# Sliding-window attention ahead of an expert layer: a longer pipeline (four stages instead of three between the scores and their use), a second transposed-probability buffer, a third value buffer, and another order on DVE

## The chip, the cores and the metric

One core of a Trainium2 chip. The time is the device time of one execution, in microseconds (us). Engines: PE (TensorE, matrix products), DVE (VectorE), ACT (ScalarE), POOL (GpSimd), SP (SyncE, which here only issues DMAs). Each works its own instructions in order and meets the others at semaphores.

## The reference

```python
B, H, S, D = 4, 8, 576, 64            # q, k, v
mask = (rel >= 0) & (rel < 64)        # each query sees itself and 63 keys before it
attn = softmax(where(mask, q @ k.T / 8, -1e9))
x = (attn @ v)  ->  (B*S, H*D) = (2304, 512)
P = exp(x @ w_gate - max); 8 rounds of row and column normalisation   # 2304 x 8
out = sum over 8 experts e of P[:, e] * (relu(x @ w1[e]) @ w2[e])       # w1 512x1024, w2 1024x512
```

## The kernel before, in words

**Attention** works on 16 pairs of heads (`NP`), numbered p. Of a pair, 9 blocks of 64 queries are treated at once, each against 128 keys (its own 64 and the 64 before). The stages of a pair, with the short names used below:

- S(p), PE, `scores` L343: 36 small products into the PSUM area `ps_s`.
- own(p), ACT, `own` L601: copies the own-block half of the scores to `sc`, one of three buffers.
- merge(p), DVE, `merge`: L923 puts the previous-block half over it where the mask says so, and lets PE have `ps_s` again (`scores_taken`); L926 takes the row maximum.
- shift(p), POOL, L825: subtracts the maximum. exp(p), ACT, L596.
- soften(p), DVE, L931 and L933: row sums and their reciprocals. weigh(p), POOL, L833: `probs`, two buffers.
- T(p), PE, `transpose` L355, into the PSUM area `ps_t`. turned(p), DVE, L917: masks it into `p_t`, one buffer.
- v_shift(p), ACT, L607: builds the "block before" rows of V in `v_win`, two buffers. M(p), PE, `mix` L366.
- x_copy(p), ACT, L614 and L617: copies x out of PSUM, and for p < 8 rounds parts of it to `xv_hi`. x_part_rests(p), DVE, L941: the rounding rest `xv_lo`.

The order of all of it is written out by hand. In turn p of the loop PE runs S(p), M(p-3), T(p-2); DVE turned(p-3), merge(p), soften(p-1), x_part_rests(p-3); ACT exp(p-1), own(p), x_copy(p-3), v_shift(p-2); POOL shift(p), weigh(p-1), and in some turns a piece of preparation for the expert layer (`w1_first_rest`, `sums_first`, `sums_last`, `w1_rest`, `x_sum`). ACT has two such pieces: `w1_first` and `w1_split`.

**After the loop** come four first-layer products of expert 0, `plain(0)` to `plain(3)`, each of 12 matmuls (L467 to L469), with the last mixes and transposes between them, then the gate products (L375). Before the first S(0) PE multiplies zeros 12 times (L531).

**The expert layer** is 96 steps of seven-product 2x2 block multiplication for the first layer (L445 to L449) and 2 x 6 x 3 matmuls for the second (L486 to L488), with DVE, ACT and POOL splitting operands into a rounded part and a rest. The change leaves it as it is.

Of the kernel before, what the change touches and what calls it, by code (L numbers as in the profile page):

```python
# [12 lines left out]
P = 128  # L13
# [17 lines left out]
QKR = 3  # L31
WARM = 12
# [34 lines left out]
def build(nc, qk, v, w_gate, w1, w2, consts, out):  # L67
    with ExitStack() as ctx:
# [17 lines left out]
        p1 = sb(ctx, "p1", [P, HT])  # L86
        u2 = sb(ctx, "u2", [P, HT])
        u3 = sb(ctx, "u3", [P, HT])
        u4 = sb(ctx, "u4", [P, HT])

        wg = sb(ctx, "wg", [P, KT, GC])
        logits = sb(ctx, "logits", [P, NT, E])
        prob = sb(ctx, "prob", [P, NT, E])
# [3 lines left out]
        max_diag = sb(ctx, "max_diag", [P, P])  # L97
# [6 lines left out]
        with ExitStack() as att:  # L104
            qk_buf = sb(att, "qk_buf", [P, QKR, QK])
            v_win = sb(att, "v_win", [P, 2, QB, P])
            sc = sb(att, "sc", [P, SCR, QB, WINDOW])
# [4 lines left out]
            soft_inv = sb(att, "soft_inv", [P, SCR, QB])  # L112
        warm = p_t[:].rearrange("p i c -> p (i c)").bitcast(mybir.dt.bfloat16)
# [5 lines left out]
        w2_lo += [sb(ctx, "w2_lo1", [P, 2, DM], F32R)]  # L119

# [8 lines left out]
        ps_t = ps[:, 1536:1536 + QB * P].rearrange("p (i c) -> p i c", i=QB)  # L129
        x_at = 7 * 512 - 5 * WINDOW  # L130
# [20 lines left out]
        v_loaded = [sem(f"v_loaded{i}") for i in range(2)]  # L151
# [112 lines left out]
        def _(sp):  # L264
# [6 lines left out]
            def load_v(p):  # L271

                if p >= 2:
                    sp.wait_ge(x_done, p - 1)
                sp.dma_start(v_win[WINDOW:P, p % 2, :, :], v[p]).then_inc(v_loaded[p % 2], 16)
# [15 lines left out]
            load_v(0)  # L291
            load_w1(0, 0, 0)
            load_v(1)
            for p in range(NP):
                if p + QKR < NP:
                    load_qk(p + QKR)
                if p >= 3:
                    load_v(p - 1)
                if p == 3:
                    sp.dma_start(wg[:], w_gate).then_inc(gate_loaded, 16)  # L300
                if p == 3:
# [32 lines left out]
        def _(pe):  # L334
            def scores(p):
                pe.wait_ge(qk_loaded[p % QKR], (p // QKR + 1) * 16)
                wait(pe, scores_taken, p)
                for i in range(QB):

                    at = 0 if i else WINDOW  # L340
                    for h in range(2):
                        c = slice(h * D, (h + 1) * D)
                        last = nc.tensor.matmul(ps_s[c, i, at:KEYS],  # L343
                                                qk_buf[c, p % QKR, S + i * WINDOW:S + (i + 1) * WINDOW],
                                                qk_buf[c, p % QKR, max(i - 1, 0) * WINDOW:(i + 1) * WINDOW],
                                                start=True, stop=True)
                last.then_inc(scores_done, 1)
# [184 lines left out]
            pe.wait_ge(pads_set, 2)  # L532
# [34 lines left out]
        def _(act):  # L567
# [25 lines left out]
            def exp(p):  # L593
                act.wait_ge(shifted, p + 1)
                e = sc[:, p % SCR, :, :]
                nc.scalar.activation(e, e, ACT.Exp, scale=float(D) ** -0.5).then_inc(exp_done, 1)  # L596

            def own(p):
                act.wait_ge(scores_done, p + 1)
                wait(act, probs_ready, p - SCR + 1)  # L600
                nc.scalar.copy(sc[:, p % SCR, :, :], ps_s[:, :, WINDOW:KEYS]).then_inc(own_taken, 1)  # L601

            def v_shift(p):

                act.wait_ge(v_loaded[p % 2], (p // 2 + 1) * 16)
                wait(act, x_done, p - 1)
                nc.scalar.copy(v_win[0:WINDOW, p % 2, 1:QB, :], v_win[WINDOW:P, p % 2, 0:QB - 1, :])\  # L607
                  .then_inc(v_shifted, 1)
# [11 lines left out]
            def p1_copy(n, slot):  # L620
                act.wait_ge(prod_done, n * PRODUCTS + (P1 + 1 - PRODUCTS))
                wait(act, u2_done, n + -1)
                nc.scalar.copy(p1[:], bank[slot]).then_inc(p1_out, 1)
# [77 lines left out]
            for p in range(NP):  # L701
# [9 lines left out]
                if p == 9:  # L711
                    w1_split(1, 1, 0)
                if p == 14:
                    x_split(0, P6)
            x_split(0, P7)
            v_shift(NP - 2)
            x_copy(NP - 3)
            exp(NP - 1)
            plain_relu(0)
            w2_split(16, 0, 0)  # L720
            x_split(0, P5)
            v_shift(NP - 1)
            plain_relu(1)
            x_copy(NP - 2)
            x_split(0, P4)
            plain_relu(2)
            x_copy(NP - 1)
            plain_relu(3)
# [22 lines left out]
        def _(pool):  # L751
# [76 lines left out]
            def weigh(p):  # L828
# [4 lines left out]
                nc.gpsimd.tensor_tensor(probs[:, p % 2, :, :, :], sc[:, k, :, :].unsqueeze(2).to_broadcast(both),  # L833
# [6 lines left out]
            for p in range(NP):  # L840
# [3 lines left out]
                if p in (5, 6):  # L844
                    w1_first_rest(p - 5)
                if p == 7:
                    sums_first(1, 16)
                if p == 8:
                    sums_last(1, 1)
                if p == 9:  # L850
                    x_sum(0, T1)
                if p == 10:
                    w1_rest(1, 1, 0, 2)
                if p == 11:
                    w1_rest(1, 1, 2, 4)
                if p == 12:
                    x_sum(0, T2)
                if p == 13:
                    w1_rest(1, 1, 4, 7)
                if p == 14:  # L860
                    x_sum(0, T3)
            weigh(NP - 1)
            x_rest(0, P6, 1)
            w2_rest(0, 0)
# [48 lines left out]
        def _(dve):  # L913
            def turned(p):
                dve.wait_ge(transposed, p + 1)
                wait(dve, x_done, p)
                nc.vector.tensor_tensor(p_t[:], ps_t, seen.unsqueeze(1).to_broadcast([P, QB, P]), ALU.mult)\  # L917
                  .then_inc(p_t_ready, 1)

            def merge(p):  # L920
                k = p % SCR
                dve.wait_ge(own_taken, p + 1)
                nc.vector.copy_predicated(sc[:, k, :, :], take_before.unsqueeze(1).to_broadcast([P, QB, WINDOW]),  # L923
                                          ps_s[:, :, 0:WINDOW]).then_inc(scores_taken, 1)
                dve.wait_ge(scores_taken, p + 1)
                nc.vector.tensor_reduce(row_max[:, k, :], sc[:, k, :, :], AX_X, ALU.max).then_inc(max_done, 1)  # L926

            def soften(p):
                k = p % SCR
                dve.wait_ge(exp_done, p + 1)  # L930
                nc.vector.tensor_reduce(soft_sum[:, k, :], sc[:, k, :, :], AX_X, ALU.add).then_inc(sum_done, 1)  # L931
# [19 lines left out]
            def add_u2(n, slot):  # L951
                dve.wait_ge(prod_done, n * PRODUCTS + (P6 + 1 - PRODUCTS))
                dve.wait_ge(p1_out, n)
                nc.vector.tensor_tensor(u2[:], bank[1 - slot], p1[:], ALU.add).then_inc(u2_done, 1)  # L954

            def add_u3(n, slot):
                dve.wait_ge(prod_done, n * PRODUCTS + (P7 + 1 - PRODUCTS))
                dve.wait_ge(u2_done, n)
                nc.vector.tensor_tensor(u3[:], bank[1 - slot], u2[:], ALU.add).then_inc(u3_done, 1)

            def add_c22(n, slot):
                dve.wait_ge(prod_done, n * PRODUCTS + (P5 + 1 - PRODUCTS))
                nc.vector.tensor_tensor(u4[:], bank[slot], u2[:], ALU.add).then_inc(u4_done, 1)  # L963
                dve.wait_ge(u3_done, n)
                dve.wait_ge(u4_done, n)
                nc.vector.tensor_tensor(bank[slot], bank[slot], u3[:], ALU.add).then_inc(c_done, 1)

            def add_c21(n, slot):
                dve.wait_ge(prod_done, n * PRODUCTS + (P4 + 1 - PRODUCTS))
                nc.vector.tensor_tensor(bank[1 - slot], bank[1 - slot], u2[:], ALU.add).then_inc(c_done, 1)  # L970

            def add_c12(n, slot):
                dve.wait_ge(prod_done, n * PRODUCTS + (P3 + 1 - PRODUCTS))
                nc.vector.tensor_tensor(bank[slot], bank[slot], u4[:], ALU.add).then_inc(c_done, 1)  # L974
# [106 lines left out]
            nc.vector.memset(ps_s[:, 0, 0:WINDOW], NEG).then_inc(pads_set, 1)  # L1081
            dve.wait_ge(const_loaded, 16)
            for p in range(NP):
                if p >= 3:
                    turned(p - 3)
                merge(p)
                if p:
                    soften(p - 1)
                if p >= 3:
                    x_part_rests(p - 3)  # L1090
            turned(NP - 3)
            soften(NP - 1)
# [76 lines left out]
```

## Time and profile before

| | us |
|---|---|
| median of 3 runs | 1604.66 (1604.3 to 1604.78) |
| the profiled execution | 1606.06 |
| its span, first to last instruction | 1604.2 |
| PE busy, share of the span | 1583.3 (99%) |
| DVE, ACT, POOL busy | 694.2, 544.8, 990.4 |
| first gate product on PE | 100.98 after the span's start |
| 16 loads of Q and K, 576 KB each, to landing | 6.4 (median) |
| 16 loads of V, 288 KB each, to landing | 4.3 (median) |

The profiled execution took 1.86 us more than its span (what lies around it) and 1.40 us more than the median. A busy PE in this table need not be working at its peak; whether it is held up is seen in its idle time and in what ended it.

### The profile page before, as it was taken

How to read it: one execution, taken by the hardware profiler on the slowest of the kernel's cores; microseconds unless marked ns; L12 is line 12 of the kernel's file. 1: busy time of each engine (PE TensorE's matmuls, PEld its weight loads, DVE VectorE, ACT ScalarE, POOL GpSimd, SP SyncE). 2: the span in 40 equal slices, each digit the busy share in tenths (PEclk: the TensorE clock that was granted, in tenths of full speed). 3: DMA queues.
4: the chain of work that ended last, by engine and by line, in shares of the span. 5: the costliest groups of instructions: out<-in, count | busy, mean ns of one | idle time of the engine just before them, and what ended most of it. 6: DMA issues, size and time to landing. Idle time of an engine off the chain costs nothing.

```text
span 1604.2 us, 24055 instructions
## 1 busy us (share of the span) xinstructions
PE 1583.3 (99%) x8886; PEld 1420.8 (89%) x8886; DVE 694.2 (43%) x1261; ACT 544.8 (34%) x785; POOL 990.4 (62%) x642
## 2 busy tenths in 40 slices
PE   7899999999999999999999999999999999999999
PEld 6789888989899888989989898998989889898988
DVE  6744543443443434434434434434344344344343
ACT  4643242323333342333323233333323333332331
POOL 4985656556565976656565565878556565655652
PEclk9999999999999999999999999999999999999999
DMA  7621212121211213121121212113121212212111
GB/s 218 177 73 67 79 54 79 53 79 52 78 62 69 78 52 119 53 79 61 70 78 52 78 52 78 60 71 118 53 79 53 78 57 73 78 52 78 52 65 39
DMA packets 34159, 120.44 MB, mean 75 GB/s; under 512 B 3904, under 2 KB 4160, under 8 KB 34112
## 3 DMA queue, kind: packets, MB, share of 16 engines
q1 hardware_dynamic: 34112, 119.80, 21.9%
q8 instruction: 31, 0.51, 0.1%
q14 instruction: 16, 0.13, 0.0%
HBM read 115.06 MB, written 4.72 MB: 75 GB/s over the span
## 4 chain that ended last, share of the span: by engine, by line
PE 94%; POOL 4%; issue 1%; DVE 1%; ACT 0%; POOLq 0%; DVEq 0%
PE ps L488 17%; PE ps L487 17%; PE ps L486 16%; PE ps L449 14%; PE ps L445 14%; PE ps L447 14%; POOL probs L833 2%; POOL sc L825 1%; PE ps L343 0%; POOL t_raw L814 0%; PE ps L531 0%; PE ps L355 0%; POOL w_lo L791 0%; DVE x_raw L990 0%; PE ps L366 0%
## 5 line engine op out<-in xcount | busy, mean ns | idle before, releaser
L791 POOL TENSOR_TENSOR w_lo<-w_raw,w_hi 128x1792 fp32r<-128x1792 f32 (+2 forms) x97 | 386.5, 3985 | 540.2 <-ACT w_hi L571 540.2
L626 ACT ACTIVATE h_hi<-ps 128x384 fp32r<-128x384 f32 x384 | 186.5, 492 | 872.3 <-DVE ps L974 434.0
L488 PE MATMUL ps<-w_hi,h_lo 128*128 128x512 f32 x1152 | 454.1, 394 | 0.0
L487 PE MATMUL ps<-w_lo,h_hi 128*128 128x512 f32 x1152 | 453.1, 393 | 0.0
L486 PE MATMUL ps<-w_hi,h_hi 128*128 128x512 f32 x1152 | 451.5, 392 | 0.0
L449 PE MATMUL ps<-xv_hi,w_lo 128*128 128x384 f32 x1330 | 445.8, 335 | 0.0
L445 PE MATMUL ps<-xv_hi,w_hi 128*128 128x384 f32 x1330 | 444.8, 334 | 0.7 <-DVE h_lo L948 0.7
L447 PE MATMUL ps<-xv_lo,w_hi 128*128 128x384 f32 x1330 | 444.3, 334 | 0.0
L948 DVE SCALAR_TENSOR_TENSOR h_lo<-ps,h_hi 128x384 fp32r<-128x384 f32 x384 | 205.9, 556 | 266.8 <-ACT h_hi L626 257.9
L445 PEld LDWEIGHTS ps<-xv_hi,w_hi 128*128 128x128 f32 x1330 | 249.7, 188 | 17.9 <-DVE h_lo L948 2.0
L447 PEld LDWEIGHTS ps<-xv_lo,w_hi 128*128 128x128 f32 x1330 | 249.7, 188 | 16.7
L488 PEld LDWEIGHTS ps<-w_hi,h_lo 128*128 128x128 f32 x1152 | 216.0, 187 | 48.0
L449 PEld LDWEIGHTS ps<-xv_hi,w_lo 128*128 128x128 f32 x1330 | 249.7, 188 | 0.0
L487 PEld LDWEIGHTS ps<-w_lo,h_hi 128*128 128x128 f32 x1152 | 216.0, 188 | 34.4
L486 PEld LDWEIGHTS ps<-w_hi,h_hi 128*128 128x128 f32 x1152 | 216.2, 188 | 34.0
L798 POOL TENSOR_TENSOR w_lo<-w_raw,w_hi 128x1024 fp32r<-128x1024 f32 x96 | 231.0, 2406 | 14.0 <-ACT w_hi L582 14.0
L571 ACT CAST w_hi<-w_raw 128x1792 fp32r<-128x1792 f32 x95 | 161.5, 1700 | 5.6 <-POOL w_raw L773 5.5
L974 DVE TENSOR_TENSOR ps<-ps,u 128x384 f32<-128x384 f32 x95 | 53.8, 567 | 234.7 <-PE ps L449 234.7
L954 DVE TENSOR_TENSOR u<-ps,p 128x384 f32<-128x384 f32 x95 | 53.0, 558 | 158.3 <-PE ps L449 158.3
L990 DVE SCALAR_TENSOR_TENSOR x_raw<-ps,prob,x_raw 128x512 f32<-128x512 f32 x126 | 93.9, 748 | 59.0 <-PE ps L488 58.1
L963 DVE TENSOR_TENSOR u<-ps,u 128x384 f32<-128x384 f32 x95 | 53.0, 558 | 137.8 <-PE ps L449 137.8
L582 ACT CAST w_hi<-w_raw 128x1024 fp32r<-128x1024 f32 x96 | 99.7, 1039 | 0.0
(87 smaller groups left out, 961.4 us busy)
## 6 DMA issues: line engine op xcount, KB each, us to landing
w_raw<-w SPq DMA_DIRECT2D x192, 512.0 KB, 3.9
qk_buf<-qk SPq DMA_DIRECT2D x16, 576.0 KB, 6.4
v_win<-v SPq DMA_DIRECT2D x16, 288.0 KB, 4.3
out<-x_raw SPq DMA_DIRECT2D x18, 256.0 KB, 4.3
const_sb<-consts SPq DMA_DIRECT2D x1, 176.0 KB, 3.6
wg<-w_gate SPq DMA_DIRECT2D x1, 64.0 KB, 5.1
```

The lines of the kernel that those rows point to most:

```text
L445: nc.tensor.matmul(o, w1_hi[:, slot, c], xv_hi[:, at, kk, :], start=(opens and kk == 0), stop=False, skip_group_check=not opens)
L447: nc.tensor.matmul(o, w1_hi[:, slot, c], xv_lo[:, at, kk, :], start=False, stop=False, skip_group_check=not opens)
L449: last = nc.tensor.matmul(o, w1_lo[:, slot, c], xv_hi[:, at, kk, :], start=False, stop=(kk == 1), skip_group_check=not opens)
L486: nc.tensor.matmul(ps_y[t], h_hi[slot][:, f, c], w2_hi[slot][:, f, :], start=opens, stop=False)
L487: nc.tensor.matmul(ps_y[t], h_hi[slot][:, f, c], w2_lo[slot][:, f, :], start=False, stop=False)
L488: last = nc.tensor.matmul(ps_y[t], h_lo[slot][:, f, c], w2_hi[slot][:, f, :], start=False, stop=closes)
L571: nc.scalar.copy(w1_hi[:, slot, :], w1_raw[:, slot, BLK:RAW]).then_inc(w1_hi_ready, 1)
L582: nc.scalar.copy(w2_hi[slot][:].rearrange("p f d -> p (f d)"), w2_raw[:, slot, :])\
L626: nc.scalar.activation(h_hi[slot][:, f, half * HT:(half + 1) * HT], o, ACT.Relu)\
L791: last = nc.gpsimd.tensor_tensor(w1_lo[:, slot, c], w1_raw[:, slot, (lo + 1) * BLK:(hi + 1) * BLK], w1_hi[:, slot, c].bitcast(F32), ALU.su ...
L798: nc.gpsimd.tensor_tensor(w2_lo[slot][:].rearrange("p f d -> p (f d)"), w2_raw[:, slot, :], w2_hi[slot][:].rearrange("p f d -> p (f d)").b ...
L948: nc.vector.scalar_tensor_tensor(h_lo[slot][:, f, c], o, 0.0, h_hi[slot][:, f, c].bitcast(F32), ALU.max, ALU.subtract).then_inc(h_ready, 1)
```

## The change

- `v_win` gets three buffers (`VR`), and `load_v(p)` waits for M(p-3) in place of M(p-2).
- `p_t` gets a second buffer for odd pairs, `us`, which is the memory of `p1`, `u2`, `u3` of the expert layer, idle until then. turned(p) waits for M(p-2) in place of M(p-1).
- To make room, `sc` has two buffers of its own, and the third lies in a part of `w1_raw` that is unused until the expert layer. `logits`, `prob` and `max_diag` lie elsewhere. (In the trace `us` and `w_raw` then stand where `p_t` and `sc` stood.)
- S(1) goes to `ps_t`, so that it need not wait for merge(0); S(2) waits for merge(0), S(3) for merge(2).
- In turn p PE runs S(p), T(p-3), M(p-4). DVE runs soften(p-1), merge(p), turned(p-3), x_part_rests(p-4). ACT runs exp(p-1), own(p), v_shift(p-3), x_copy(p-4). One more mix and transpose lie behind the loop.
- The pieces for the expert layer sit one turn later or so: `w1_first` at turn 5, `w1_split` at 10; on POOL, turns 6 to 11, 12, 13 and 14, the third `x_sum` behind the loop. The load of w1 moves from the start to turn 3.

```diff
             def transpose / mix / attend (PE)
-                wait(pe, scores_taken, p)
+                wait(pe, scores_taken, {1: 0, 2: 1}.get(p, p))
-                        last = nc.tensor.matmul(ps_s[c, i, at:KEYS],
+                        last = nc.tensor.matmul(ps_of[p][c, i, at:KEYS],
...
                 if p < NP:
                     scores(p)
-                if p >= 3:
-
-                    wait(pe, x_taken, p - 3)
-                    wait(pe, x_part_lo, parts_in(p - 3))
-                    mix(p - 3)
-                if 2 <= p < NP + 2:
-                    transpose(p - 2)
+                if 3 <= p < NP + 3:
+                    transpose(p - 3)
+                if p >= 4:
+                    wait(pe, x_taken, p - 4)
+                    wait(pe, x_part_lo, parts_in(p - 4))
+                    mix(p - 4)
...
             plain(0)
             attend(NP)
+            attend(NP + 1)
             plain(1)
-            attend(NP + 1)
+            attend(NP + 2)
             plain(2)
-            attend(NP + 2)
+            attend(NP + 3)
             plain(3)
```

```diff
                 dve.wait_ge(transposed, p + 1)
-                wait(dve, x_done, p)
-                nc.vector.tensor_tensor(p_t[:], ps_t, ...)
+                wait(dve, x_done, p - 1)
+                nc.vector.tensor_tensor(p_ts[p % 2], ps_t, ...)
...
             for p in range(NP):
+                if p:
+                    soften(p - 1)
+                merge(p)
                 if p >= 3:
                     turned(p - 3)
-                merge(p)
-                if p:
-                    soften(p - 1)
-                if p >= 3:
-                    x_part_rests(p - 3)
-            turned(NP - 3)
+                if p >= 4:
+                    x_part_rests(p - 4)
             soften(NP - 1)
+            turned(NP - 3)
```

```diff
             def load_v(p):
-                if p >= 2:
-                    sp.wait_ge(x_done, p - 1)
+                if p >= VR:
+                    sp.wait_ge(x_done, p - VR + 1)
...
                 own(p)
                 if p >= 3:
-                    x_copy(p - 3)
-                if p >= 2:
-                    v_shift(p - 2)
-                if p == 4:
+                    v_shift(p - 3)
+                if p >= 4:
+                    x_copy(p - 4)
+                if p == 5:
                     w1_first()
-                if p == 9:
+                if p == 10:
                     w1_split(1, 1, 0)
```

How PE's instructions stand at the start. Before, from S(2) (first two rows) to S(4):

```order
L343 MATMUL ps<-qk_buf 64x64 x2
L343 MATMUL ps<-qk_buf 64x128 x16
L355 MATMUL ps<-const_sb,probs 128x128 x9
L343 MATMUL ps<-qk_buf 64x64 x2
L343 MATMUL ps<-qk_buf 64x128 x16
L366 MATMUL ps<-p_t,v_win 64x64 x18
L355 MATMUL ps<-const_sb,probs 128x128 x9
L343 MATMUL ps<-qk_buf 64x64 x2
L343 MATMUL ps<-qk_buf 64x128 x16
```

In the changed kernel (L351 is S, L363 T, L374 M), from S(2) to S(5):

```order
L351 MATMUL ps<-qk_buf 64x64 x2
L351 MATMUL ps<-qk_buf 64x128 x16
L351 MATMUL ps<-qk_buf 64x64 x2
L351 MATMUL ps<-qk_buf 64x128 x16
L363 MATMUL ps<-const_sb,probs 128x128 x9
L351 MATMUL ps<-qk_buf 64x64 x2
L351 MATMUL ps<-qk_buf 64x128 x16
L363 MATMUL ps<-const_sb,probs 128x128 x9
L374 MATMUL ps<-p_t,v_win 64x64 x18
L351 MATMUL ps<-qk_buf 64x64 x2
L351 MATMUL ps<-qk_buf 64x128 x16
```

T(0) stood between S(2) and S(3) and now stands behind S(3); M(0) has moved from behind S(3) to behind S(4) and T(1).

DVE's turn 7 before, which is turned(4), merge(7), soften(6), x_part_rests(4), and the turned(5) that opens the next:

```order
L917 TENSOR_TENSOR p_t<-ps,const_sb 128x1152
L923 COPY_PREDICATED sc<-const_sb,ps 128x576
L926 TENSOR_REDUCE row_max<-sc 128x9
L931 TENSOR_REDUCE soft_sum<-sc 128x9
L933 RECIPROCAL soft_inv<-soft_sum 128x9
L941 TENSOR_TENSOR xv_lo<-ps,xv_hi 128x192
L917 TENSOR_TENSOR p_t<-ps,const_sb 128x1152
```

DVE's turn 8 in the changed kernel, which is soften(7), merge(8), turned(5), x_part_rests(4), and the sums that open the next:

```order
L940 TENSOR_REDUCE soft_sum<-sc 128x9
L942 RECIPROCAL soft_inv<-soft_sum 128x9
L932 COPY_PREDICATED w_raw<-const_sb,ps 128x576
L935 TENSOR_REDUCE row_max<-w_raw 128x9
L926 TENSOR_TENSOR us<-ps,const_sb 128x1152
L950 TENSOR_TENSOR xv_lo<-ps,xv_hi 128x192
L940 TENSOR_REDUCE soft_sum<-w_raw 128x9
```

The sums of the pair before stood behind the merge and now stand ahead of it; turned stood ahead of the merge and now stands behind it.

## Rows read from the trace of the kernel before

**Rows 1.** The chain that ended last, from 0 to 130 us, by line.
```profile
by line: POOL probs L833 21.0%; POOL sc L825 12.2%; issue 11.0%; PE ps L343 3.6%; POOL t_raw L814 3.4%; PE ps L445 3.1%; PE ps L531 3.1%; PE ps L486 3.1%; PE ps L449 3.0%; PE ps L447 2.9%; PE ps L488 2.9%; PE ps L487 2.8%; PE ps L355 2.7%; 
```

**Rows 2.** Windows: stretch and length, then each engine's busy us.
```profile
60.00:80.00 20.00, 17.16 (x323) 15.50 (x320) 15.45 (x23) 12.34 (x21) 18.02 (x12) 1.00 0.53 139
120.00:140.00 20.00, 20.00 (x103) 18.06 (x102) 9.71 (x23) 5.49 (x9) 9.83 (x7) 1.00 0.24 87
```

**Rows 3.** Waits of PE, 19 to 101 us: total us, times, longest.
```profile
PE ps L366 <- DVE p_t L917: 5.5, 8, 1.3
```

**Rows 4.** Timeline of PE: start, length, line, tiles, count, idle before.
```profile
14.69 2.08 PE L343 MATMUL ps<-qk_buf 64*64 64x64 f32 x36 [2.01 <-DVE sc L923]
...
19.88 2.08 PE L343 MATMUL ps<-qk_buf 64*64 64x64 f32 x36
21.89 1.27 PE L366 MATMUL ps<-p_t,v_win 128*64 128x64 f32 x36
23.09 1.20 PE L355 MATMUL ps<-const_sb,probs 128*128 128x128 f32 x9
24.22 2.08 PE L343 MATMUL ps<-qk_buf 64*64 64x64 f32 x36
...
80.29 2.08 PE L343 MATMUL ps<-qk_buf 64*64 64x64 f32 x36
...
85.07 0.42 PE L467 MATMUL ps<-xv_hi,w_hi 128*128 128x384 f32 x1
...
87.34 1.27 PE L366 MATMUL ps<-p_t,v_win 128*64 128x64 f32 x36
...
100.98 0.63 PE L375 MATMUL ps<-x_raw,wg 128*32 128x512 f32 x3
```

**Rows 5.** Timeline of all engines, 11 to 16 us: one round of the softmax stages.
```profile
11.32 1.15 POOL L825 TENSOR_TENSOR sc<-sc,row_max 128x576 f32<-128x576 f32 x1 [10.27 <-DVE row_max L926]
12.51 0.68 ACT L596 ACTIVATE sc<-sc 128x576 f32<-128x576 f32 x1 [2.96 <-POOL sc L825]
...
13.75 0.79 DVE L923 COPY_PREDICATED sc<-const_sb,ps 128x576 f32<-128x576 uint32 x1 [2.51 <-ACT sc L601]
14.58 0.75 DVE L926 TENSOR_REDUCE row_max<-sc 128x9 f32<-128x576 f32 x1
...
15.41 1.15 POOL L825 TENSOR_TENSOR sc<-sc,row_max 128x576 f32<-128x576 f32 x1 [2.94 <-DVE row_max L926]
```

**Rows 6.** Timeline of ACT and DVE, 89 to 91 us: exp(15) and its sums.
```profile
89.32 0.68 ACT L596 ACTIVATE sc<-sc 128x576 f32<-128x576 f32 x1
...
90.03 0.76 DVE L931 TENSOR_REDUCE soft_sum<-sc 128x9 f32<-128x576 f32 x1 [3.06 <-ACT sc L596]
```

**Rows 7.** Timeline of DVE, 24 to 27 us, without idle time between.
```profile
23.54 0.76 DVE L926 TENSOR_REDUCE row_max<-sc 128x9 f32<-128x576 f32 x1
24.21 0.74 DVE L931 TENSOR_REDUCE soft_sum<-sc 128x9 f32<-128x576 f32 x1
24.98 0.21 DVE L933 RECIPROCAL soft_inv<-soft_sum 128x9 f32<-128x9 f32 x1
25.11 0.76 DVE L941 TENSOR_TENSOR xv_lo<-ps,xv_hi 128x384 fp32r<-128x384 f32 x2
25.79 1.35 DVE L917 TENSOR_TENSOR p_t<-ps,const_sb 128x1152 f32<-128x1152 f32 x1
```

**Rows 8.** Timeline, 54 to 58 us: a weigh and an extra piece on POOL, `w1_split` on ACT.
```profile
55.22 2.12 POOL L833 TENSOR_TENSOR probs<-sc,soft_inv 128x1152 f32<-128x1152 f32 x1
56.02 1.69 ACT L571 CAST w_hi<-w_raw 128x1792 fp32r<-128x1792 f32 x1
...
57.29 1.82 POOL L814 TENSOR_TENSOR t_raw<-x_raw 128x768 f32<-128x768 f32 x1
```

**Rows 9.** Timeline of PE, 2 to 9 us: the zero products, then S(0).
```profile
2.14 4.02 PE L531 MATMUL ps<-p_t 128*128 128x384 bf16 x12 [2.14 <-DVE p_t L1079]
6.09 2.77 PE L343 MATMUL ps<-qk_buf 64*64 64x64 f32 x36
```

More of the change, by code:

```diff
@@ L31 @@
 QKR = 3
+VR = 3
 WARM = 12
@@ L85, in build @@
         w2_raw = sb(ctx, "w2_raw", [P, 2, 2 * DM])
[L86 to L89, printed above, removed]
+        us = sb(ctx, "us", [P, 4, HT])
+        p1, u2, u3, u4 = (us[:, i, :] for i in range(4))
         wg = sb(ctx, "wg", [P, KT, GC])
-        logits = sb(ctx, "logits", [P, NT, E])
-        prob = sb(ctx, "prob", [P, NT, E])
         col_part = sb(ctx, "col_part", [P, E])
@@ L112, in build @@
             soft_inv = sb(att, "soft_inv", [P, SCR, QB])
+        v_bufs = [v_win[:, i, :, :] for i in range(VR)]
+        p_ts = [p_t[:], us[:].rearrange("p r t -> p (r t)")[:, 0:QB * P].rearrange("p (i c) -> p i c", i=QB)]
+        sc_of = [sc[:, i, :, :] for i in range(SCR - 1)]
+        sc_of += [w1_raw[:, 0, 4 * BLK:4 * BLK + QB * WINDOW].rearrange("p (i c) -> p i c", i=QB)]
         warm = p_t[:].rearrange("p i c -> p (i c)").bitcast(mybir.dt.bfloat16)
@@ L119, in build @@
         w2_lo += [sb(ctx, "w2_lo1", [P, 2, DM], F32R)]
+        logits = sb(ctx, "logits", [P, NT, E])
+        prob = sb(ctx, "prob", [P, NT, E])
+        max_diag = sb(ctx, "max_diag", [P, P])
         take_before = const_sb[:, 0:WINDOW].bitcast(mybir.dt.uint32)
@@ L129, in build @@
         ps_t = ps[:, 1536:1536 + QB * P].rearrange("p (i c) -> p i c", i=QB)
+        ps_of = [ps_t if p == 1 else ps_s for p in range(NP)]
         x_at = 7 * 512 - 5 * WINDOW
@@ L150, in build @@
         qk_loaded = [sem(f"qk_loaded{i}") for i in range(QKR)]
-        v_loaded = [sem(f"v_loaded{i}") for i in range(2)]
+        v_loaded = [sem(f"v_loaded{i}") for i in range(VR)]
         v_shifted = sem("v_shifted")
@@ L296, in _ @@
                     load_qk(p + QKR)
-                if p >= 3:
+                if p < VR:
+                    load_v(p)
+                if p > VR:
                     load_v(p - 1)
@@ L365, in mix @@
                         c = slice(h * D, (h + 1) * D)
-                        last = nc.tensor.matmul(ps_x[c, i * WINDOW:(i + 1) * WINDOW], v_win[:, p % 2, i, c],
-                                                p_t[:, i, c], start=True, stop=True)
+                        last = nc.tensor.matmul(ps_x[c, i * WINDOW:(i + 1) * WINDOW], v_bufs[p % VR][:, i, c],
+                                                p_ts[p % 2][:, i, c], start=True, stop=True)
                 last.then_inc(x_done, 1)
@@ L600, in own @@
                 wait(act, probs_ready, p - SCR + 1)
-                nc.scalar.copy(sc[:, p % SCR, :, :], ps_s[:, :, WINDOW:KEYS]).then_inc(own_taken, 1)
+                nc.scalar.copy(sc_of[p % SCR], ps_of[p][:, :, WINDOW:KEYS]).then_inc(own_taken, 1)
             def v_shift(p):
-                act.wait_ge(v_loaded[p % 2], (p // 2 + 1) * 16)
-                wait(act, x_done, p - 1)
-                nc.scalar.copy(v_win[0:WINDOW, p % 2, 1:QB, :], v_win[WINDOW:P, p % 2, 0:QB - 1, :])\
+                act.wait_ge(v_loaded[p % VR], (p // VR + 1) * 16)
+                wait(act, x_done, p - VR + 1)
+                nc.scalar.copy(v_bufs[p % VR][0:WINDOW, 1:QB, :], v_bufs[p % VR][WINDOW:P, 0:QB - 1, :])\
                   .then_inc(v_shifted, 1)
@@ L705, in _ @@
                 if p >= 3:
-                    x_copy(p - 3)
-                if p >= 2:
-                    v_shift(p - 2)
-                if p == 4:
+                    v_shift(p - 3)
+                if p >= 4:
+                    x_copy(p - 4)
+                if p == 5:
                     w1_first()
-                if p == 9:
+                if p == 10:
                     w1_split(1, 1, 0)
-                if p == 14:
-                    x_split(0, P6)
-            x_split(0, P7)
+            v_shift(NP - 3)
+            exp(NP - 1)
+            plain_relu(0)
+            x_split(0, P6)
+            x_copy(NP - 4)
             v_shift(NP - 2)
             x_copy(NP - 3)
-            exp(NP - 1)
-            plain_relu(0)
+            plain_relu(1)
+            v_shift(NP - 1)
             w2_split(16, 0, 0)
+            x_split(0, P7)
+            x_copy(NP - 2)
             x_split(0, P5)
[L722 to L725, printed above, removed]
             plain_relu(2)
             x_copy(NP - 1)
+            x_split(0, P4)
             plain_relu(3)
@@ L843, in _ @@
                     weigh(p - 1)
-                if p in (5, 6):
-                    w1_first_rest(p - 5)
-                if p == 7:
+                if p in (6, 7):
+                    w1_first_rest(p - 6)
+                if p == 8:
                     sums_first(1, 16)
-                if p == 8:
+                if p == 9:
                     sums_last(1, 1)
-                if p == 9:
+                if p == 10:
                     x_sum(0, T1)
-                if p == 10:
+                if p == 11:
                     w1_rest(1, 1, 0, 2)
-                if p == 11:
+                if p == 12:
                     w1_rest(1, 1, 2, 4)
-                if p == 12:
-                    x_sum(0, T2)
                 if p == 13:
@@ L915, in turned @@
                 dve.wait_ge(transposed, p + 1)
-                wait(dve, x_done, p)
-                nc.vector.tensor_tensor(p_t[:], ps_t, seen.unsqueeze(1).to_broadcast([P, QB, P]), ALU.mult)\
+                wait(dve, x_done, p - 1)
+                nc.vector.tensor_tensor(p_ts[p % 2], ps_t, seen.unsqueeze(1).to_broadcast([P, QB, P]), ALU.mult)\
                   .then_inc(p_t_ready, 1)
@@ L930, in soften @@
                 dve.wait_ge(exp_done, p + 1)
-                nc.vector.tensor_reduce(soft_sum[:, k, :], sc[:, k, :, :], AX_X, ALU.add).then_inc(sum_done, 1)
+                nc.vector.tensor_reduce(soft_sum[:, k, :], sc_of[k], AX_X, ALU.add).then_inc(sum_done, 1)
                 dve.wait_ge(sum_done, p + 1)
@@ L953, in add_u2 @@
                 dve.wait_ge(p1_out, n)
-                nc.vector.tensor_tensor(u2[:], bank[1 - slot], p1[:], ALU.add).then_inc(u2_done, 1)
+                nc.vector.tensor_tensor(u2, bank[1 - slot], p1, ALU.add).then_inc(u2_done, 1)
             def add_u3(n, slot):
```

47 lines of the change are left out of this document (22 added, 25 removed).

## The prediction

> **What bounds the kernel now.** I read the windows first. In the expert layer PE is busy for 20.00 of 20 us; between 60 and 80 us, inside attention, for 17.16 [rows 2]. The change touches attention alone, so what it can move is the moment at which the gate products start, 100.98 us [rows 4]; PE is the limit from there on, and every microsecond gained or lost there should arrive at the end unchanged. Next the chain: over the first 130 us a third of it is weigh and shift on POOL (21.0% and 12.2%) [rows 1], so attention is bound by a round trip through several engines. The waits of PE say where that shows: 8 mixes waited 5.5 us in all for `p_t` [rows 3]. The timeline gives PE's own need: S starts at 19.88, M at 21.89, T at 23.09, the next S at 24.22, with no idle time [rows 4], so S costs 2.01, M 1.20, T 1.13, together 4.34 a pair. From S(4) at 24.22 to `plain(0)` at 85.07 there are 12 turns [rows 4] in 60.85 us, 5.07 each. At 4.34 they would take 52.1. So 8.8 us at most stand to be had there.
>
> **The change, part by part.**
>
> *Second `p_t`, third V, one more stage.* M(p-4) needs turned(p-4), made a whole turn earlier, and V stands in one of three buffers, so that its load starts a turn further ahead of its use. The 5.5 us of waits [rows 3] should go.
>
> *DVE's new order.* This is the part with a price. Soften(p-1) now stands ahead of merge(p), so a ring closes through every pair: shift, exp, sums, reciprocals, merge, maximum, next shift. From starts: shift to exp 12.51 - 11.32 = 1.19, merge to maximum 14.58 - 13.75 = 0.83, maximum to shift 15.41 - 14.58 = 0.83 [rows 5]; exp to sums 90.03 - 89.32 = 0.71 [rows 6]; sums to reciprocal 0.77, reciprocal to the next instruction 0.13 [rows 7]. Sum: 1.19 + 0.71 + 0.77 + 0.13 + 0.83 + 0.83 = **4.46 us a pair**. Before, own(p) alone lay between exp and merge and the ring took 15.41 - 11.32 = 4.09 [rows 5]. So the new floor is 4.46, set by the ring, not PE's 4.34. While shift and exp run, DVE is free from the end of the maximum for about 2.05 us (0.83 + 1.19 + 0.71 from its start, less the 24.21 - 23.54 = 0.67 that it holds DVE [rows 7]); turned (1.35) and the largest x_part_rests (0.68, the step from 25.11 to 25.79) fit with 2.03 [rows 7]. I cost them at nothing; were that cover gone, each 0.1 us would cost 0.4 over the four turns that have the large rests.
>
> *The start.* shift(0) starts at 11.32 as before. S(1) no longer waits for merge(0), which saves nothing: own(1) stands behind exp(0) on ACT anyway. shift(1) comes 0.4 later than the 15.41 of before. S(p+1) starts 0.72 ahead of shift(p) (14.69 against 15.41 [rows 4, 5]).
>
> *Extra pieces.* POOL needs shift and weigh, about 1.16 + 2.07 = 3.23, in a turn (57.29 - 55.22 = 2.07 [rows 8]). A piece of 1.82 us [rows 8] makes it 5.03 and so adds 0.57 to the ring. Four are of that length: turns 6, 10, 13 and 14 (the last delays only shift(15)). The two pairs of short sums (turns 8, 9), some 1.4 to 1.5 together, add 0.2 to 0.3 each. ACT's `w1_first` at turn 5, about 1.0, stands between x_copy(1) and exp(5), where ACT has some 0.7 to spare: 0.3. `w1_split`, 1.69 [rows 8], overlaps turn 10's POOL piece: nothing more. Up to shift(14): 3 x 0.57 + 0.45 + 0.3 = 2.4.
>
> So shift(14) at 11.32 + 14 x 4.46 + 2.4 = 76.2 and S(15) at 75.5, against 80.29 [rows 4]: 4.8 us earlier.
>
> *The end.* PE then has S(15), four T, five M (one more than before) and four `plain` at 2.2 (85.07 to 87.34 less its wait [rows 4]): 2.0 + 4.6 + 6.0 + 8.8 = 21.4. Shift(15) is at 76.2 + 5.0 = 81.2; turned(13) stands behind soften(15) and ends at 81.2 + 1.19 + 0.71 + 0.90 + 1.35 = 85.4, and T(14) waits for it 0.9 us, the M(12) before it ending at 84.5. M(15) waits for x_copy(14), which is behind `w2_split` on ACT, but that ends at about 93.8, ahead of PE at 94.4. The gate starts at 75.5 + 21.4 + 0.9 = 97.8, **3.2 us earlier**. POOL's last rests come 2.5 earlier and had slack. Loads: V is issued a turn or more ahead of need and lands in 4.3; Q and K have 11 us for 6.4.
>
> *A hole on PE.* S(2) ends near 12.9 (S(1) from 8.9, S(2) behind it), and T(0), which used to fill the hole, stands behind S(3), which needs merge(2): 11.32 + 2 x 4.46 - 0.72 = 19.5. PE stands still for 6.6 us, where before no hole after the zero products was above 2.01 [rows 4]. What idleness does to it can be seen at the start: the zero products of 384 columns took 4.02 / 12 = 0.335 us each [rows 9], while the 12 products of `plain(0)`, as wide, took 87.34 - 85.07 = 2.27, 0.19 each [rows 4]: the first is the 1.2 GHz level, the second the 2.4 GHz one (the clock column of the windows reads 1.00 throughout [rows 2], and it reads so early on too, so here the spacing must tell). S(0) took 2.77 [rows 9] against the 2.08 of later ones [rows 4], so it began at the low level and ended at the high one: at half speed for about 1.4 us, PE came up some 5.4 us after its first product.
>
> The Trainium skill ("TensorE: Matmul & The Clock Gate", section "What's actually happening") says that the slow level is the default and that idleness brings it back. The zero products agree; no row of before shows a fall after work. By that rule the hole costs the 1.5 us worked out below, without it nothing.
>
> Price if the level has fallen by S(3) and returns about 5.4 us later: S(3) takes almost double, some 3.8 and not 2.0, own(3), due at 22.0, waits to 23.3, and merge(3) comes 1.0 late. T(0) takes twice as long, PE runs half a microsecond behind the ring, so x_copy(1) and `w1_first` end later and exp(5) slips a further 0.5. Together 1.5. The bounds: 0 if it doesn't fall, and 1.8 more for each further S at the low level.
>
> **The forecast.** 1604.66 - 3.2 + 1.5 = **1603.0**. (Of the profiled execution, 1606.06 would become 1604.4; I apply the difference to the median.) A change under 0.2%, 3.2 us, can't be told from none by a measurement of this kernel.
>
> **The rivals.**
> - *PE keeps its clock*: 1604.66 - 3.2 = 1601.5. For it: 2 us holes did no harm. Against: this one is three times as long.
> - *The low level stays a little longer*, one or two more S: +1.8 to +3.6 on the forecast, 1604.8 to 1606.6, so no change.
> - *The low level stays for the whole loop*, slower than before. At half speed a pair needs up to 2 x 4.34 = 8.7 us against 4.46, over 12 turns 50 us: 1653. It decides if S, T and M with the holes of the first turns are too little activity to raise the clock. The trace shows it only kept by such work, never raised by it alone: the rise came behind twelve full-width products. Against it: at half speed PE would be busy without a break. The Trainium skill (same page, "Part 4: PE-mode transpose") says that transposes don't count as activity in the same way; no row here tests that.
> - *The ring is looser than I think*: the extra pieces hide, up to 2.4 us more gain, 1599.1 to 1601.
> - *The change does not do what it says* because the rest of the gain is lost at the end (ACT or POOL late for the last mixes): 1604 to 1605, the small change of the forecast again.
>
> **Chances.** Forecast 0.50 (own range 1602.0 to 1604.3); clock kept 0.24; low a little longer 0.12; low for good 0.05; looser ring 0.05; end eats it 0.04. Faster by over 0.2% (below 1601.45): half of clock kept and the looser ring and a little of the forecast, 0.20. Slower by over 0.2% (above 1607.9): 0.07. Within: 0.73. The range reaches from 1600.6 (part of the looser ring) to 1605.7 (part of the low level's further stay).
>
> **What would show it.** S starts from turn 4 on spaced by 4.4 to 4.6 and 5.0 where POOL has a long piece; PE's waits on `p_t` and V gone, in their place S waiting for the merge; a hole of some 6.6 us between S(2) and S(3); S(3) of about 3.7 us if the clock fell, 2.1 if not; the gate at 99.3 (97.8 if not). Behind the gate nothing should differ. I am wrong if soften(p-1) doesn't hold up merge(p), if Q, K or V land late at the faster pace, or if the expert layer's own windows change length.

## The result, and the profile after

| | before | changed |
|---|---|---|
| median of 5 runs, us | 1604.78 | 1595.88 |
| ratio, 95% interval | | 0.9945 (0.9934 to 0.9957) |
| profiled execution, span | 1604.2 | 1594.6 |
| first gate product | 100.98 | 98.58 |
| from there to the end of the span | 1503.2 | 1496.0 |

The change made the kernel 8.9 us faster by the medians, where 1.7 had been forecast. The two profiled spans differ by 9.6 us: attention, the part that was argued about, came out 2.4 us shorter in this pair of profiles (further ones below give less), and 7.2 us were gained behind the gate, in code that the change doesn't touch and where no difference was forecast.

**Attention.** The waits of PE in the changed kernel (total us, times, longest), from 19 to 101 us; the waits of the mixes for `p_t` of [rows 3] are gone, and so are those of the transposes for the weights from POOL:

```profile
PE ps L351 <- DVE w_raw L932: 8.0, 3, 6.8
PE ps L363 <- DVE us L926: 1.0, 1, 1.0
PE ps L475 <- DVE sc L932: 0.5, 1, 0.5
PE ps L351 <- DVE sc L932: 0.4, 1, 0.4
```

In the kernel before, in the same stretch:

```profile
PE ps L355 <- POOL probs L833: 3.5, 4, 2.0
```

Of the 8.0, one wait of 6.8 is the hole ahead of S(3). The 1.0 is T(14) waiting for turned(13), forecast at 0.9. The timeline of PE shows the hole and what follows it:

```profile
6.09 6.39 PE L351 MATMUL ps<-qk_buf 64*64 64x64 f32 x108
19.25 3.89 PE L351 MATMUL ps<-qk_buf 64*64 64x64 f32 x36 [6.76 <-DVE w_raw L932]
23.07 1.74 PE L363 MATMUL ps<-const_sb,probs 128*128 128x128 f32 x9
24.80 2.08 PE L351 MATMUL ps<-qk_buf 64*64 64x64 f32 x36
...
75.53 2.08 PE L351 MATMUL ps<-qk_buf 64*64 64x64 f32 x36
...
98.58 0.63 PE L383 MATMUL ps<-x_raw,wg 128*32 128x512 f32 x3
```

S(3), L351 at 19.25, takes 3.89 us and S(4) 2.08; S(15) starts at 75.53 (75.5 had been worked out before the price of the clock). The windows of PE, whose third number from the end is the granted clock, agree:

```profile
14.00:16.00 2.00, 0.00 (x0) 1.00 1.01 281
16.00:18.00 2.00, 0.00 (x0) 0.85 0.99 233
18.00:20.00 2.00, 0.75 (x10) 0.50 0.98 205
20.00:22.00 2.00, 2.00 (x22) 0.50 0.22 48
22.00:24.00 2.00, 2.00 (x17) 0.50 0.01 5
24.00:26.00 2.00, 2.00 (x30) 0.95 0.88 247
```

PE had done nothing since about 12.5. The clock fell to half, 1.2 GHz, between 16 and 18, inside the hole, and was back at 2.4 GHz soon after 24, some 5 us after S(3) began. The softmax ring, POOL's shift of pairs 0 to 2 (answering to [rows 5]):

```profile
11.13 1.15 POOL L835 TENSOR_TENSOR sc<-sc,row_max 128x576 f32<-128x576 f32 x1 [9.97 <-DVE row_max L935]
...
15.55 1.15 POOL L835 TENSOR_TENSOR sc<-sc,row_max 128x576 f32<-128x576 f32 x1 [3.27 <-DVE row_max L935]
...
19.97 1.15 POOL L835 TENSOR_TENSOR w_raw<-w_raw,row_max 128x576 f32<-128x576 f32 x1 [1.20 <-DVE row_max L935]
```

15.55 - 11.13 = 19.97 - 15.55 = 4.42 us a pair; 4.46 had been summed. By the same trace the next shift comes 5.55 us later, behind the S(3) at half clock.

**The expert layer.** The windows of PE from 200 to 1500 us, the kernel before first, then the changed one:

```profile
200.00:1500.00 1300.00, 1299.32 (x6496) 1.00 0.20 70
```

```profile
200.00:1500.00 1300.00, 1299.02 (x6529) 1.00 0.20 70
```

PE is busy without a break in both, at the full clock in both, and yet gets through 33 more matmuls in the same 1300 us. A step has 78 matmuls (42 + 36), so it lasts 1300 x 78 / 6496 = 15.61 us before and 15.53 after. The 0.5% on 1496 us is the 7 us. The busy share and the clock show nothing here; only the spacing does. A run of six second-layer products before, between two runs of L445 to L449:

```profile
1005.15 0.40 PE L486 MATMUL ps<-w_hi,h_hi 128*128 128x512 f32 x1
1005.39 0.40 PE L487 MATMUL ps<-w_lo,h_hi 128*128 128x512 f32 x1
1005.62 0.40 PE L488 MATMUL ps<-w_hi,h_lo 128*128 128x512 f32 x1
1005.86 0.39 PE L486 MATMUL ps<-w_hi,h_hi 128*128 128x512 f32 x1
1006.08 0.39 PE L487 MATMUL ps<-w_lo,h_hi 128*128 128x512 f32 x1
1006.31 0.39 PE L488 MATMUL ps<-w_hi,h_lo 128*128 128x512 f32 x1
1006.54 0.33 PE L445 MATMUL ps<-xv_hi,w_hi 128*128 128x384 f32 x1
```

In the changed kernel, the first of a run of eighteen, behind L457:

```profile
1001.87 0.39 PE L494 MATMUL ps<-w_hi,h_hi 128*128 128x512 f32 x1
1002.10 0.39 PE L495 MATMUL ps<-w_lo,h_hi 128*128 128x512 f32 x1
1002.32 0.39 PE L496 MATMUL ps<-w_hi,h_lo 128*128 128x512 f32 x1
1002.55 0.39 PE L494 MATMUL ps<-w_hi,h_hi 128*128 128x512 f32 x1
1002.78 0.39 PE L495 MATMUL ps<-w_lo,h_hi 128*128 128x512 f32 x1
1003.00 0.39 PE L496 MATMUL ps<-w_hi,h_lo 128*128 128x512 f32 x1
1003.23 0.39 PE L494 MATMUL ps<-w_hi,h_hi 128*128 128x512 f32 x1
```

Six products take 1006.54 - 1005.15 = 1.39 us before and 1003.23 - 1001.87 = 1.36 after. The first three before are the slow ones: 0.71 against 0.68 us. That is no accident of one place. Worked out from the starts of all runs of eighteen between 200 and 1500 us in the two traces (83 in each), the mean steps from one product to the next are 238, 233, 236, 224, 231, 236, 228, 232 and 231 ns before, and 227 from the tenth on; in the changed kernel they are 226 to 228 from the first (in both, the last step, back to a product with xv, is longer: 237 and 235). So before, PE needs about nine products behind a switch from xv to w2 until it runs at the short spacing.

### The profile page after: what moved, and what is told of

It is laid out like the page before. It is cut to its first block, busy times and chain, and to the rows that moved or that the text cites. A ratio compares the mean times of both kernels' runs of the same rounds, so it can differ in the third digit from the quotient of the medians.

```text
span 1594.6 us, 24053 instructions
## 1 busy us (share of the span) xinstructions
PE 1577.8 (99%) x8886; PEld 1426.9 (89%) x8886; DVE 693.6 (43%) x1262; ACT 543.7 (34%) x785; POOL 991.3 (62%) x642
## 4 chain that ended last, share of the span: by engine, by line
PE 92%; POOL 6%; DVE 1%; issue 1%; ACT 1%; DVEq 0%; POOLq 0%; ACTq 0%
PE ps L496 16%; PE ps L494 16%; PE ps L495 16%; PE ps L457 14%; PE ps L455 14%; PE ps L453 14%; POOL probs L843 2%; POOL xv_lo L829 1%; POOL sc L835 1%; POOL w_lo L801 1%; POOL w_raw L835 0%; POOL w_lo L808 0%; PE ps L539 0%; PE ps L374 0%; ACT w_hi L580 0%
## 5 line engine op out<-in xcount | busy, mean ns | idle before, releaser
L457 PE MATMUL ps<-xv_hi,w_lo 128*128 128x384 f32 x1330 | 448.3, 337 | 0.0
L495 PE MATMUL ps<-w_lo,h_hi 128*128 128x512 f32 x1152 | 448.2, 389 | 0.0
L457 PEld LDWEIGHTS ps<-xv_hi,w_lo 128*128 128x128 f32 x1330 | 249.4, 188 | 0.0
L983 DVE TENSOR_TENSOR ps<-ps,us 128x384 f32<-128x384 f32 x95 | 53.8, 566 | 232.3 <-PE ps L457 232.3
L963 DVE TENSOR_TENSOR us<-ps,us 128x384 f32<-128x384 f32 x95 | 53.0, 557 | 157.3 <-PE ps L457 157.3
L972 DVE TENSOR_TENSOR us<-ps,us 128x384 f32<-128x384 f32 x95 | 52.9, 557 | 136.6 <-PE ps L457 136.6
```

The costliest lines, as they stand in the source:

```text
L457: last = nc.tensor.matmul(o, w1_lo[:, slot, c], xv_hi[:, at, kk, :], start=False, stop=(kk == 1), skip_group_check=not opens)
L495: nc.tensor.matmul(ps_y[t], h_hi[slot][:, f, c], w2_lo[slot][:, f, :], start=False, stop=False)
```

## Experiments

Two theories stood for the 7 us. *Placement*: the change takes `logits`, `prob` and `max_diag` (576 + 576 + 512 bytes per partition) away from ahead of the operands of the second layer, so that these lie 1664 bytes lower. *Clock*: the fall and return of PE's clock leaves its stream in another rhythm. The address of `w2_hi0`, as allocated when the kernel is built, is 175328 before and 173664 after, that of `h_hi0` 183520 and 181856; all buffers of w2 and h (`hi` and `lo`, 0 and 1) have in each kernel the same remainder by 256, **224 before, 96 after**. xv and w1 have 128 in both.

**e1, placement alone.** In the kernel before:

```diff
-        logits = sb(ctx, "logits", [P, NT, E])
-        prob = sb(ctx, "prob", [P, NT, E])
...
-        max_diag = sb(ctx, "max_diag", [P, P])
...
         w2_lo += [sb(ctx, "w2_lo1", [P, 2, DM], F32R)]
+        logits = sb(ctx, "logits", [P, NT, E])
+        prob = sb(ctx, "prob", [P, NT, E])
+        max_diag = sb(ctx, "max_diag", [P, P])
```

> The kernel before with only logits, prob and max_diag moved, so that the operands of the expert layer lie at the addresses of the changed kernel. Placement theory: the second-layer matmuls come at the shorter spacing (about 6529 matmuls in 1300 us of the expert layer, mean 389 to 392 ns) and the time is about 1604.8 - 7 = 1597.5. Clock theory (the fall and return of the clock leaves PE's stream in another rhythm): nothing changes, 6496 matmuls in 1300 us, 1604.8. Attention as before in both, gate at 101.0.

Measured: 1597.26 us, ratio 0.9954 (0.9938 to 0.9971). The windows of PE:

```profile
200.00:1500.00 1300.00, 1299.00 (x6530) 1.00 0.20 70
```

Three buffers that the products of the expert layer's steps don't read (`max_diag` is read by one small product, L498), moved without any other edit, bring 7.2 us by the medians. With them moves all that is declared behind them, w2 and h too.

**e2, the hole filled.** In the changed kernel:

```diff
                     scores(p)
+                if p == 2:
+                    for i in range(36):
+                        nc.tensor.matmul(ps_y[5][:, 0:HT], warm[:, 0:P], warm[:, 0:HT], start=True, stop=True)
```

> The changed kernel with 36 more products of zeros on PE between S(2) and T(0)'s place, so that the hole is filled and the clock need not fall; the filler is extra work without a use. Clock theory: no fall, S(3) takes 2.1 and not 3.9 us, the gate starts about 1 us earlier (97.6), and the expert layer goes back to the slow rhythm of before (6496 in 1300 us), so about 1595.9 - 1 + 7 = 1602. Placement theory: the expert layer stays at 6529 in 1300 us and the time is about 1595.

Measured: 1594.78 us, 0.9941 (0.9925 to 0.9958). 6527 matmuls in the 1300 us. The windows of PE over the hole, then its timeline, with S(3) and T(0) at the full clock, and the gate:

```profile
16.00:18.00 2.00, 2.00 (x13) 1.00 0.96 300
18.00:20.00 2.00, 1.70 (x34) 1.00 0.06 16
```

```profile
18.32 2.08 PE L351 MATMUL ps<-qk_buf 64*64 64x64 f32 x36 [0.30 <-DVE w_raw L935]
20.33 1.20 PE L363 MATMUL ps<-const_sb,probs 128*128 128x128 f32 x9
...
96.51 0.63 PE L383 MATMUL ps<-x_raw,wg 128*32 128x512 f32 x3
```

No fall of the clock, and the short rhythm stays: the clock theory falls. The gate comes 98.58 - 96.51 = 2.1 us earlier. But the first shift on POOL also starts earlier in this execution, at 10.19 and not 11.13, ahead of hole and filler. From the first shift to the gate it is 86.3 us against 87.4, 1.1 less, and all of it lies between shift(2) and shift(3), 4.43 us against 5.55. So the hole costs 1.1 us. By the medians e2 is 1.1 us below the changed kernel too, but the intervals of the two ratios (0.9941 and 0.9945) don't separate them.

**e3, a hole in the kernel before.**

```diff
-                pe.wait_ge(probs_ready, p + 1)
+                pe.wait_ge(probs_ready, max(p + 1, 2))
```

> The kernel before with T(0) waiting for weigh(1), which makes a hole of about 6 us on PE behind S(2). Clock theory: the clock falls for a while, the start of the gate comes 4 to 6 us later than 101.0, but the expert layer runs at the short spacing (6529 in 1300 us): 1604.8 + 5 - 7 = 1603. Placement theory: the expert layer stays at 6496 in 1300 us and the time is about 1610.

Measured: 1610.5 us, 1.0037 (1.0023 to 1.0052). The windows of PE, early and in the expert layer:

```profile
20.00:22.00 2.00, 0.00 (x0) 0.65 0.17 67
22.00:24.00 2.00, 1.43 (x7) 0.50 0.00 0
...
200.00:1500.00 1300.00, 1299.34 (x6494) 1.00 0.20 70
```

The clock fell in a hole of 6.1 us here too, and the long rhythm stayed. Fall of the clock and rhythm have nothing to do with each other, in either direction.

**e4, DVE's order undone.** In the changed kernel:

```diff
-                if p:
-                    soften(p - 1)
                 merge(p)
+                if p:
+                    soften(p - 1)
                 if p >= 3:
                     turned(p - 3)
```

> The changed kernel with merge(p) ahead of soften(p-1) on DVE, as before. Ring theory: the start has a ring of 4.1 and not 4.42 us, later PE's own 4.4 sets the pace, so S(15) and the gate come 0.5 to 1.5 us earlier than 98.58, the time about 1595. Rival: DVE holds soften back so that weigh and T come late; gate at 99 or later, 1596 or more. The rhythm of the expert layer should be that of the changed kernel if either placement or the clock sets it.

Measured: 1595.87 us, 0.9945 (0.9928 to 0.9962); gate at 98.29, 6530 matmuls. The waits of PE, 15 to 100 us:

```profile
PE ps L351 <- DVE w_raw L932: 6.3, 2, 6.1
PE ps L363 <- DVE p_t L926: 2.2, 4, 0.8
PE ps L363 <- DVE us L926: 2.0, 4, 0.8
```

The ring is open (the first two shifts are 4.08 and 4.10 us apart in this trace), but turned(p-3) now stands later on DVE, and T waits 4.2 us for `ps_t` to be read. By the times the two orders cost the same. From the first shift to the gate the profile has 86.7 us against the 87.4 of the changed kernel, so the old order may be up to 0.8 us better; the times don't show it.

**e5, only the first pair of w2 buffers moved.** In the kernel before, `logits`, `prob` and `max_diag` are declared behind `w2_lo0`: `w2_hi0` and `w2_lo0` lie at 96 by 256, h and the second w2 pair stay at 224.

```diff
         w2_lo = [sb(ctx, "w2_lo0", [P, 2, DM], F32R)]
+        logits = sb(ctx, "logits", [P, NT, E])
+        prob = sb(ctx, "prob", [P, NT, E])
+        max_diag = sb(ctx, "max_diag", [P, P])
```

> The kernel before with logits, prob and max_diag moved behind w2_lo0: w2_hi0 and w2_lo0 (moving operand of the second layer in every other step) lie 1664 bytes lower as in the changed kernel, h_hi, h_lo and the other w2 buffers lie where they did. If the address of the moving operand w2 sets the rhythm: every other step is short, half the gain, about 6513 matmuls in 1300 us, 1601. If the address of the loaded operand h sets it: 6496 and 1604.5. If something else that moved does (ones, constants, logits, prob): 6529 and 1597.

Measured: 1608.51 us, 1.0023 (1.0011 to 1.0034), 6481 matmuls. Slower than before, which none of the three expected outcomes was. That is 1300 x 78 / 6481 = 15.65 us a step on average; if the steps on the second buffers keep their 15.61, those with w2 at 96 and h at 224 take about 15.68. The starts in this trace bear that out: between 250 and 1500 us the steps alternate between 15.60 and 15.68 us (medians), the long ones on the first buffers, where in the kernel before both kinds take 15.60 (the 15.61 is an average with a few longer steps). So w2's place counts, and not by itself.

**e6, e7, e8, e10: the placement of e1 with 32, 128, 512 and 256 bytes more.**

```diff
+        pad = sb(ctx, "pad", [P, 8])       # e7: 32, e8: 128, e10: 64 values
         w2_hi = [sb(ctx, "w2_hi0", [P, 2, DM], F32R)]
```

> The placement of the first experiment with 32 bytes more ahead of w2_hi0, so that w2 and h start at multiples of 64 and 128 bytes (128 above a multiple of 256), as xv and w1 do. If what matters is the place within 64 or 128 bytes: a third rhythm, perhaps shorter than 15.52 us a step (up to 36 x 3 ns = 0.1 us a step, 1588 in all). If only bit 7 of the address counts: 6496, 1604. If neither: 6529, 1597.

> The placement of the first experiment with 128 bytes more ahead of w2_hi0: w2 and h lie 224 above a multiple of 256, as in the kernel before, but 1536 bytes lower than there. If the place within 256 bytes sets the rhythm: slow again, 6496, 1604.5. If the distance in larger units (1536 bytes) does: 6529, 1597.

> The placement of the first experiment with 512 bytes more: the place within 512 bytes is unchanged (96). If the place within 256 or 512 bytes sets the rhythm: 6529, 1597. If larger units do: something else.

> The placement of the first experiment with 256 bytes more: the place within 256 bytes is the same (96), that within 512 differs (352). If only the place within 256 bytes counts: 6530 and 1597. If that within 512: something else, 6496 or fewer.

| | w2 and h by 256 | by 512 | matmuls in 1300 us | us | ratio (95%) |
|---|---|---|---|---|---|
| e6, +32 | 128 | 128 | 6494 | 1605.32 | 1.0005 (0.9994 to 1.0017) |
| e7, +128 | 224 | 224 | 6496 | 1604.53 | 0.9998 (0.9987 to 1.0010) |
| e8, +512 | 96 | 96 | 6530 | 1596.86 | 0.9953 (0.9933 to 0.9972) |
| e10, +256 | 96 | 352 | 6530 | 1597.76 | 0.9955 (0.9939 to 0.9971) |

128 bytes take the whole gain away; 256 and 512 leave it. Of the places tried, what counts is the remainder by 256. A stricter view is the part of each profile from the first gate product to the end of the span, which leaves attention out: 1495.9 to 1496.0 us in all seven profiles with both at 96 (the changed kernel, e1, e2, e4, e8, e10, e12), 1503.1 to 1503.3 in all four with both at 224 (before, e3, e7, e9), 1503.7 at 128 (e6). Being a multiple of 128, like xv and w1, doesn't help (e6).

**e9, the changed kernel with 128 unused bytes.** The same pad of 32 values in the changed kernel: w2 and h are back at 224.

> The changed kernel with 128 unused bytes ahead of w2_hi0, so that w2 and h lie 224 and not 96 bytes above a multiple of 256; nothing else differs. Placement theory: the expert layer takes the rhythm of the kernel before (6496 matmuls in 1300 us), the gate starts at 98.6 as in the changed kernel, and the time is 1604.8 - 2.4 = 1602.4. If placement explained only a part: between 1596 and 1602.

Measured: 1603.02 us, 0.9989 (0.9979 to 0.9999). The windows of PE and the gate:

```profile
200.00:1500.00 1300.00, 1299.32 (x6497) 1.00 0.20 70
```

```profile
97.81 0.63 PE L384 MATMUL ps<-x_raw,wg 128*32 128x512 f32 x3
```

This is the change as it was argued about, with w2 and h at their old remainder (1536 bytes lower than before, a distance that cost nothing in e7): 2.0 us faster than before.

**e11, the fourth corner.** e1 with pads so that w2 lies at 224 and h at 96.

```diff
+        pad = sb(ctx, "pad", [P, 32])
         w2_hi = [sb(ctx, "w2_hi0", [P, 2, DM], F32R)]
         w2_lo = [sb(ctx, "w2_lo0", [P, 2, DM], F32R)]
+        pad2 = sb(ctx, "pad2", [P, 32])
...
+        pad3 = sb(ctx, "pad3", [P, 32])
         w2_hi += [sb(ctx, "w2_hi1", [P, 2, DM], F32R)]
```

> The first experiment with w2 at 224 above a multiple of 256 and h at 96; the fourth corner beside both at 96 (15.52 us a step), both at 224 (15.60) and w2 at 96 with h at 224 (15.68). If what counts is h's place alone, plus a price for a mixed pair: 15.6 or more. If the two add up, from w2 -0.08 to +0.08 in the one case: the four can't be additive with both 224 below the mixed one unless this corner is the shortest, 15.44 (6560 in 1300 us, 1589). If they must be alike: 15.6 to 15.7, 1605 to 1609.

Measured: 1616.55 us, 1.0074 (1.0054 to 1.0094), on two runs. The windows of PE:

```profile
200.00:1500.00 1300.00, 1299.43 (x6443) 1.00 0.19 69
```

| us a step | h at 96 | h at 224 |
|---|---|---|
| w2 at 96 | 15.53 | 15.68 (from e5) |
| w2 at 224 | 15.74 | 15.61 |

Both mixed pairs are worse than both alike; the two operands act together. By their remainders e11 and e7 differ only in h (and in scratch space of attention), and e11 is 12 us longer. Its slow products are of another kind: in its runs of eighteen the steps go 229, 237, 229, 237 ns to the end and never settle.

**e12, filler and merge first together**, the edits of e2 and e4 in the changed kernel.

> The changed kernel with both the filler products and merge(p) ahead of soften(p-1) on DVE. Alone the filler brought the gate to 96.5 and the order to 98.3 (from 98.6). If they add: the gate at 96.2 and 1594.5. If merge first only helps while PE is late after the fall of the clock: 96.5 to 97, 1595.

Measured: 1594.90 us, 0.9937 (0.9920 to 0.9953), gate at 97.41. By the times not better than e2; no sum of the two gains shows. (From the first shift, at 11.62, to the gate it is 85.8 us, 0.5 less than in e2; the late gate comes of the late start.) e2 and e12 have the lowest times of all that ran, but lie within each other's intervals, and 1.1 us below the changed kernel is less than these intervals settle.

## Why the prediction was wrong

**The step that failed** is in the first paragraph: that PE is the limit from the gate on "and every microsecond gained or lost there should arrive at the end unchanged", repeated as "Behind the gate nothing should differ". The list of parts left out one edit of the diff, that `logits`, `prob` and `max_diag` lie elsewhere, and so gave it neither a price nor a bound. e1 prices it at 7.2 us, e9 takes it back: with it undone, the changed kernel takes 1603.02 us, against 1603.0 forecast. That close a match is partly luck: the gain is known to be 0.2 to 3.4 us only, and errors inside attention offset each other, as told below. The recorded text did give a change of length in the expert layer's windows as a sign of being wrong, and that sign came. Nothing in the trace of before could have sized it, but it could have been named as an edit without a row, and the range kept open for it.

**Point by point, in attention:**

- *p_t and V, one more stage*: right. No mix waits in the changed kernel. The same stage also took away 3.5 us of waits of T for POOL, which the text didn't count.
- *The ring*: its length was right (4.42 against 4.46), and so were the extra pieces: turns 6, 10, 13 and 14 are 0.54 to 0.56 us longer than the ring in the trace of the changed kernel, 0.57 forecast. S(15) came at 75.53, which is 1.5 us ahead of the forecast with the price of the clock (77.0): S(15) starts 1.2 us ahead of shift(14) and not 0.72, the clock cost less, and the ring was a little shorter. From S(15) to the gate it took 23.05 us and not 22.3. That the longer ring is a price which the old order would save was largely wrong: e4 opens the ring, and its gate comes only 0.3 us earlier (0.8 counted from the first shift), since T then waits 4.2 us for turned.
- *The hole and the clock*: right in kind. The clock fell and came back some 5 us after S(3) began. S(3) took 3.89 (some 3.8 forecast), T(0) only 1.74, as the clock returned during or close behind it. The price was put at 1.5, 1.0 for a late merge(3) and 0.5 for a late exp(5). e2 gives 1.1: merge(3) was late by about that, and exp(5) not at all (shift(5) to shift(6) takes 4.87 us in the changed kernel and 4.85 in e2).
- *The gate*: 99.3 forecast, 98.58 found, and 97.81 in e9. The gate of one profile is a poor measure, since it moves with the first shift, which starts anywhere from 10.2 to 11.6 us: in the kernels with the attention code of before the gate lies between 98.79 and 100.98. From the first shift to the gate the changed kernel has 87.4 (87.5 in e9), the kernel before 89.7 in its own profile, and its attention code 88.0 to 88.5 in e1, e6, e7, e8, e10 and e11 and 90.0 in e5. So the 2.4 of the first two profiles is at the high end; the runs of e9 give 2.0 with an interval from 0.2 to 3.4, and the changed kernel is 1.4 below e1, which has the same places of w2 and h.
- *The rivals*: the clock neither stayed up nor stayed low. "2 us holes did no harm", said for the first rival, held for the one profile at hand and not in general: in the profile of e5, with the attention code of before and no hole above 2.01 us, the clock fell between 18 and 20 us and S(3) took 3.66 us and not 2.08 (below, the windows of PE in e5, which read 0.50 from 20 to 22). The median of the kernel before may mix both cases, too: of its 14 runs beside e9, the 6 with a mean granted clock of 1.000 have a median of 1604.1 us, the 8 with 0.999 one of 1605.4. One fall like that of e5 would lower the mean by about that much; that it is what those runs had isn't shown, as no trace of them was kept.

```profile
18.00:20.00 2.00, 2.00 (x23) 0.82 0.73 285
20.00:22.00 2.00, 2.00 (x22) 0.50 0.06 25
```

- *The range* missed because neither forecast nor rivals looked behind the gate.

**What stays open** is the mechanism of the placement effect. Shown is that w2 (streamed) and h (loaded) matter together, by their remainder by 256, and that it acts at full clock and with PE busy. With both at 224 the time is lost in the first nine or so products with w2 behind those with xv; with w2 at 224 and h at 96 (e11) it is lost all along. Why 96 suits and 128 and 224 don't was not found. Whether xv's and w1's 128 plays a part, and whether one of the places not tried (0, 32, 64, 160, 192) is better still, wasn't tried.

## What to carry to other kernels

Count moved buffers as an edit: where PE is busy all the time, a difference of 128 bytes in where its operands lie was worth 7 us in 1600 here, more than the pipeline stage that the change was about. When a change frees or adds memory, compare the time with a version in which the operands keep their old remainder (a pad is enough) before giving the gain to the code, and look at matmuls per stretch of time, since busy share and clock stay the same. A hole of 6 us on PE halved its clock here, until some 5 us after work had come back; zero products in the hole kept it up, for a gain of about 1.1 us, at the edge of what the times show. And a single event in a single profile, such as the gate, is compared best from a common point near it (here the first shift), since the start alone moved it by over 1 us.

## What was not expected of the hardware

- 33 more matmuls in 1300 us (6529 against 6496) with PE 100% busy at clock 1.00 in both, from the place of its operands by 256 bytes alone; the worst pair of places (e11) had 6443, 1.3% fewer than the best.
- Two operands at unlike places are slower than both at either like place: 15.68 and 15.74 us a step against 15.53 and 15.61.
- Places at a multiple of 128 bytes (e6, 6494) were no better than places at an odd multiple of 32 (e7, 6496).
- The same attention code, with holes of about 2 us between short bursts on PE, kept the clock in the profile of the kernel before and lost it for 3.4 us in that of e5 (0.50 in the window from 20 to 22 us).
